# Expert loop: VectorE splits its two thirds of the next second weights one block later, GpSimd keeps its third where it was

## The chip, the cores and the metric

The program runs on one core of a Trainium2 chip. The metric is the device time of one execution in microseconds (us). The engines are TensorE (PE in the profile; its weight loads are PEld), VectorE (DVE), ScalarE (ACT), GpSimd (POOL) and SyncE (SP, which here only starts DMA). A name with q behind it (DVEq) is the sequencer of that engine: register loads, branches and semaphore work.

## The reference, cut to what matters

Three stages follow each other. A linear attention with a decaying state gives 3072 token rows of 384 numbers. A dense layer pair (384 to 2048, leaky ReLU, back to 384) works on these rows. The last stage routes each row to one of 8 experts, and this is where the change lies:

```
do_compute = x @ w_skip > 0
e_idx = np.argmax(xc @ w_gate, axis=1)
for e in range(E):
    h = np.maximum(xc[mask] @ w1[e], 0.0)       # 384 -> 1024
    y[mask] = gate_w[mask, None] * (h @ w2[e])  # 1024 -> 384
out[do_compute] = xc + y
```

Everything is float32. The kernel reaches that precision by splitting each operand of a matmul in a high part (rounded to the type that TensorE reads fast) and a low part (what is left), and by adding three products: high by high, high by low, low by high.

## The kernel before, in words

Attention and dense layers fill most of the span. Then the rows are sorted by expert into blocks of 128 rows; every expert has at least one block, and an expert's rows are padded to whole blocks. A table called `plan` holds, for each block, its expert (`EXPERT`), which half of the weight buffers that expert uses (`PARITY`), a flag `FIRST` that is 1 in the first block of an expert (but 0 for the last expert, which has no successor to prepare), the number of blocks (`TOTAL`) and where the ids of the block's rows lie (`SPOT`). Each engine runs a loop over blocks of its own, unrolled four times, and reads the table at run time into registers with `value_load`.

The order on each engine in block j, by lines of the profile:

- TensorE: transposes the hidden block j (L806), then the first product of block j+1 (L779, 18 matmuls), which needs the low rows `zt_lo` of block j+1 and the low first weights `w1_lo`; the turning of the gathered rows of block j+2 (L772), which needs their gather to have landed; two register loads (L819, L820); and the second product of block j (L825, 24 matmuls), which waits at L821 for `eht_lo` and at L822 until all three thirds of `w2_lo` of this block's expert are there.
- ScalarE: high part of the transposed hidden block (`eht_hi`, L1066, two halves); if block j+1 is the first of an expert e, the high parts of w1 of e+1 (L949, three thirds); ReLU of the hidden block j+1 (L1045, L1046); high rows of block j+2 (`zt_hi`, L1041); if block j is the first of an expert e, the high parts of w2 of e+1 (L1038, three thirds), after waiting until `w2_lo` of e is complete.
- VectorE: low part of the hidden block (`eht_lo`, L1493, two halves); if block j+1 is the first of an expert, `w1_lo` of the next expert (L1508, three thirds); low rows (`zt_lo`, L1475); if block j is the first of an expert, its two thirds of `w2_lo` of the next expert (L1522); and last the result of block j (`res`, L1528), which waits for the second product of block j and frees its PSUM bank.
- GpSimd: if block j is the first of an expert, its third of `w2_lo` of the next expert (L1629); then it waits that the output of block j-1 has been written and that `res` of block j is there, copies the ids (`put`, L1637), scatters the rows to the output (L1640), and gathers the rows of block j+4 (L1599, L1602).
- SyncE: loads the raw weights of expert e into the half that expert e-2 used. The load of w1 (L488) waits for `w1_lo` of e-2, the load of w2 (L496) for all three thirds of `w2_lo` of e-2; before it goes on to the next expert it waits until both have landed.

Within an engine the order is that of the program. Between engines only semaphores order the work. In a `value_load` of a block's flag and the two that follow if it is 1, VectorE's sequencer does nothing else, though instructions issued before may still run.

Of the kernel before, what the change touches and what calls it, by code (L numbers as in the profile page):

```python
# [17 lines left out]
ALU = mybir.AluOpType  # L18
ACT = mybir.ActivationFunctionType
AX = mybir.AxisListType  # L20
F32 = mybir.dt.float32
# [11 lines left out]
E = 8  # L33
# [15 lines left out]
EW = KT * EF  # L49
PIECES = 3  # L50
PIECE = EW // PIECES
HOTS = 8
UNROLL = 4
COLS = BLOCKS + 1 + UNROLL
# [25 lines left out]
CONSTS = ALT + E  # L80


EXPERT, PARITY, FIRST, TOTAL, SPOT = 0, COLS, 2 * COLS, 3 * COLS, 3 * COLS + 1

def build(nc, rk_t, rk_nat, v_nat, w_cols, u_rows, win, wout, wout_t, gates, experts, consts, out, z_rows):
    ctx = ExitStack()
# [4 lines left out]
    with ctx:  # L91
# [3 lines left out]
        def sem(name):  # L95
            return ctx.enter_context(nc.semaphore(name))
# [76 lines left out]
        def sb4(name, shape, dt=F32):  # L173
            return sb(name, shape, dt, moe)

        raw2 = sb4("raw2", [P, 2 * EW])
        w2_hi = sb4("w2_hi", [P, 2 * EW], F32R)
        w2_lo = sb4("w2_lo", [P, 2 * EW], F32R)
# [23 lines left out]
        plan = sb4("plan", [P, SPOT + COLS], I32)  # L202
# [88 lines left out]
        s_w2_hi = sem("w2_hi")  # L291
        s_w2_lo = sem("w2_lo")
# [21 lines left out]
        s_dve_past = sem("dve_past")  # L314
# [786 lines left out]
        def _(dve):  # L1101
# [151 lines left out]
            def linked(ins):  # L1253

                ins.then_inc(s_route, 1)
                routed[0] += 1
                dve.wait_ge(s_route, routed[0])
# [193 lines left out]
            dve.tensor_scalar(below[:], eidf[:], float(E - 2), None, ALU.min)  # L1451
            dve.tensor_copy(plan[:, TOTAL:TOTAL + 1], ends[:, E - 1:E])
            linked(dve.tensor_reduce(par[:], cmp2[:], AX.X, ALU.add))
            dve.memset(plan[:, FIRST:FIRST + 1], 1)
            dve.tensor_tensor(plan[:, FIRST + 1:FIRST + COLS], below[:, 1:], below[:, 0:COLS - 1], ALU.subtract)
            dve.tensor_copy(plan[:, PARITY:PARITY + COLS], par[:]).then_inc(s_plan_done, 1)
# [15 lines left out]
            def turned_rows(par, n):  # L1472

                dve.wait_ge(s_zt_hi, n)
                dve.tensor_tensor(zt_lo[par][:].rearrange("a k t -> a (k t)"), bank[4][:, 0:DM],  # L1475
                                  zt_hi[par][:].rearrange("a k t -> a (k t)").bitcast(F32),
                                  ALU.subtract).then_inc(s_zt_lo, 1)
# [6 lines left out]
            with dve.Fori(0, (BLOCKS + 1) // UNROLL) as jj:  # L1484
                with dve.If(UNROLL * jj < blocks):
                    for u in range(UNROLL):
                        j = UNROLL * jj + u
                        with dve.If(j < blocks):

                            for half in range(2):  # L1490
                                dve.wait_ge(s_eht_hi, 2 * j + half + 1)
                                rows = slice(4 * half, 4 * half + 4)
                                dve.tensor_tensor(eht_lo[:, rows, :].rearrange("a f t -> a (f t)"),  # L1493
                                                  bank[2 + half][:],
                                                  eht_hi[:, rows, :].rearrange("a f t -> a (f t)").bitcast(F32),
                                                  ALU.subtract).then_inc(s_eht_lo, 1)

                            first = dve.value_load(plan[0:1, bass.ds(FIRST + j + 1, 1)], min_val=0, max_val=1)
                            with dve.If(first > 0):
                                e = dve.value_load(plan[0:1, bass.ds(EXPERT + j + 1, 1)], min_val=0,  # L1500
                                                   max_val=E - 1)
                                odd = dve.value_load(plan[0:1, bass.ds(PARITY + j + 1, 1)], min_val=0,
                                                     max_val=1)
                                for i in range(PIECES):
                                    cols = bass.ds((1 - odd) * EW + PIECE * i, PIECE)
                                    dve.wait_ge(s_w1_hi, PIECES * e + PIECES + i + 1)
                                    dve.sem_inc(s_dve_past, 1)
                                    dve.tensor_tensor(w1_lo[:, cols], raw1[:, cols], w1_hi[:, cols].bitcast(F32),  # L1508
                                                      ALU.subtract).then_inc(s_w1_lo, 1)

                            with dve.If(j < blocks - 2):
                                turned_rows(u % 2, j + 3)

                            first = dve.value_load(plan[0:1, bass.ds(FIRST + j, 1)], min_val=0, max_val=1)
                            with dve.If(first > 0):
                                e = dve.value_load(plan[0:1, bass.ds(EXPERT + j, 1)], min_val=0, max_val=E - 1)
                                odd = dve.value_load(plan[0:1, bass.ds(PARITY + j, 1)], min_val=0, max_val=1)
                                for i in range(1, PIECES):
                                    cols = bass.ds((1 - odd) * EW + PIECE * i, PIECE)
                                    dve.wait_ge(s_w2_hi, PIECES * e + PIECES + i + 1)  # L1520
                                    dve.sem_inc(s_dve_past, 1)
                                    dve.tensor_tensor(w2_lo[:, cols], raw2[:, cols], w2_hi[:, cols].bitcast(F32),  # L1522
                                                      ALU.subtract).then_inc(s_w2_lo, 1)

                            spot_j = dve.value_load(plan[0:1, bass.ds(SPOT + j, 1)], min_val=0, max_val=SPOTS - 1)
                            dve.wait_ge(s_ey_done, j + 1)
                            dve.wait_ge(s_res_free, j + 1)
                            dve.scalar_tensor_tensor(res[u % 2][:], bank[5 + u % 2][:, 0:DM],  # L1528
                                                     found[:, bass.ds(spot_j, 1), 1], zg[u][:],
                                                     ALU.mult, ALU.add).then_inc(s_res_done, 1)  # L1530
# [169 lines left out]
```

## Time and profile before

| what | value |
|---|---|
| median of 3 runs | 735.33 us (731.72 to 738.29) |
| the profiled execution | 734.31 us |
| its span, first to last instruction | 732.6 us |
| TensorE busy | 689.9 us, 94% of the span |
| VectorE, ScalarE, GpSimd busy | 405.9, 307.1, 105.0 us |
| mean granted TensorE clock | 0.979 of full speed |

The span is 1.7 us shorter than the execution's time. A busy share is an average over stages; which wait counts is read stage by stage. In rows of the timeline the first number is the start in us from the beginning of the span, the second the length, and the bracket at the end, if there is one, is how long the engine stood idle before it and what ended that. The blocks are numbered from 0; the expert loop of this input has 14.

### The profile page before, as it was taken

Reading aid. Unit: us, or ns where it says so; the run is one execution under the profiler, and the core shown is the slowest. Engines: PE = TensorE matmul, PEld = TensorE weight load, DVE = VectorE, ACT = ScalarE, POOL = GpSimd, SP = SyncE. Lnnn points to the kernel's source line nnn. Section 1 sums busy time; section 2 is a strip of 40 time slices with the busy share of each in tenths; the row PEclk is TensorE's granted clock in tenths of the full one; section 3 lists DMA queues with packets and bytes.
Section 4 is the critical chain, followed back from the end, with each engine's and each line's share of the span. In section 5 each row is a group of like instructions: output and inputs, shape, how many; then the busy total and the mean of one; then the engine's idle time right before and its main releaser. Section 6 shows DMA issues by size and latency. Waiting matters only on the chain.

```text
span 732.6 us, 14146 instructions
## 1 busy us (share of the span) xinstructions
PE 689.9 (94%) x4365; PEld 650.5 (89%) x4366; DVE 405.9 (55%) x839; ACT 307.1 (42%) x665; POOL 105.0 (14%) x120
## 2 busy tenths in 40 slices
PE   7977999999999999999999999999998899998973
PEld 7877999999999999999999999999994788987773
DVE  8654565755665565466466545533557352745741
ACT  4434544333444442444443344433442453646530
POOL 6330000010010001001000100100103152344321
PEclk9998999999999999999999999999998999999997
DMA  8645342312422132242204222006015762383200
GB/s 243 200 137 193 121 132 72 99 40 59 130 65 66 36 108 59 60 130 65 66 22 118 63 60 87 12 13 235 1 62 197 285 227 106 111 293 126 100 19 8
DMA packets 38681, 77.44 MB, mean 106 GB/s; under 512 B 8568, under 2 KB 26902, under 8 KB 38624
## 3 DMA queue, kind: packets, MB, share of 16 engines
q1 hardware_dynamic: 33632, 62.37, 27.4%
q10 hardware_dynamic: 2432, 9.76, 3.6%
q0 software_dynamic: 2560, 4.58, 2.0%
q8 instruction: 32, 0.52, 0.3%
q14 instruction: 25, 0.20, 0.1%
HBM read 61.09 MB, written 12.41 MB: 100 GB/s over the span
## 4 chain that ended last, share of the span: by engine, by line
PE 84%; DVE 4%; ACT 4%; issue 4%; ACTq 1%; DVEq 1%; POOL 1%; DMA 1%; POOLq 0%; SPq 0%
PE bank L687 28%; PE bank L705 26%; PE bank L825 6%; PE bank L779 5%; PE bank L569 4%; PE bank L625 3%; PE bank L620 2%; PE bank L764 2%; PE bank L638 2%; PE bank L806 1%; PE bank L663 1%; ACT w_hi L1038 1%; PE bank L607 1%; DVE h_sb L1202 1%; ACT h_sb L920 1%
## 5 line engine op out<-in xcount | busy, mean ns | idle before, releaser
L1202 DVE TENSOR_TENSOR h_sb<-h_sb,bank 128x384 f32<-128x384 f32 x128 | 70.8, 553 | 173.3 <-ACT h_sb L920 172.9
L920 ACT ACTIVATE h_sb<-bank 128x384 f32<-128x384 f32 x128 | 62.8, 491 | 246.8 <-PE bank L687 242.8
L687 PE MATMUL bank<-x_hi,win_hi 128*128 128x384 f32 x384 | 135.6, 353 | 2.7 <-DVE win_lo L1224 1.6
L705 PE MATMUL bank<-wout_hi,g_hi 128*128 128x394 f32 x384 | 131.7, 343 | 0.0
L705 PE MATMUL bank<-wout_lo,g_hi 128*128 128x394 f32 x384 | 131.2, 342 | 0.0
L705 PE MATMUL bank<-wout_hi,g_lo 128*128 128x394 f32 x384 | 131.2, 342 | 0.0
L687 PE MATMUL bank<-x_hi,win_lo 128*128 128x384 f32 x384 | 130.5, 340 | 0.0
L687 PE MATMUL bank<-x_lo,win_hi 128*128 128x384 f32 x384 | 130.3, 339 | 0.0
L1563 POOL DMA_INDIRECT id_list<-idgate,dst x24 | 24.2, 1007 | 480.2 <-DVE dst L1307 475.3
L1209 DVE TENSOR_TENSOR g_lo<-h_sb,g_hi 128x384 fp32r<-128x384 f32 x128 | 70.9, 554 | 33.4 <-ACT g_hi L927 32.3
L927 ACT ACTIVATE g_hi<-h_sb 128x384 fp32r<-128x384 f32 x128 | 66.7, 521 | 42.9 <-DVE h_sb L1202 40.5
L687 PEld LDWEIGHTS bank<-x_hi,win_hi 128*128 128x128 f32 x384 | 72.8, 189 | 9.4 <-issue 7.0
L687 PEld LDWEIGHTS bank<-x_lo,win_hi 128*128 128x128 f32 x384 | 73.1, 190 | 0.0
L687 PEld LDWEIGHTS bank<-x_hi,win_lo 128*128 128x128 f32 x384 | 73.0, 190 | 0.0
L705 PEld LDWEIGHTS bank<-wout_hi,g_lo 128*128 128x128 f32 x384 | 72.5, 189 | 0.0
L705 PEld LDWEIGHTS bank<-wout_hi,g_hi 128*128 128x128 f32 x384 | 72.5, 189 | 0.0
L705 PEld LDWEIGHTS bank<-wout_lo,g_hi 128*128 128x128 f32 x384 | 72.4, 188 | 0.0
L877 ACT ACTIVATE am<-const,diag 128x128 f32<-128x128 f32 x168 | 53.2, 391 | 9.6 <-PE bank L625 6.0
L825 PE MATMUL bank<-w_hi,eht_hi 128*128 x112 | 40.0, 357 | 12.0 <-DVE eht_lo L1493 9.3
L825 PE MATMUL bank<-w_hi,eht_lo 128*128 x112 | 38.9, 347 | 0.0
L825 PE MATMUL bank<-w_lo,eht_hi 128*128 x112 | 38.8, 346 | 0.0
L569 PEld LDWEIGHTS bank<-rt,kb 64*128 64x128 f32 x384 | 24.4, 193 | 14.4 <-issue 11.7
(187 smaller groups left out, 993.0 us busy)
## 6 DMA issues: line engine op xcount, KB each, us to landing
raw<-in_experts SPq DMA_DIRECT2D x32, 768.0 KB, 6.1
rkt<-in_rk_t SPq DMA_DIRECT2D x46, 192.0 KB, 3.6
rkn<-in_rk_nat SPq DMA_DIRECT2D x21, 384.0 KB, 4.1
v<-in_v_nat SPq DMA_DIRECT2D x24, 192.0 KB, 2.8
z_rows<-z_sb SPq DMA_DIRECT2D x24, 192.0 KB, 2.8
out<-z_sb SPq DMA_DIRECT2D x24, 192.0 KB, 2.8
stage<-in_win ACTq DMA_DIRECT2D x4, 768.0 KB, 4.6
stage<-in_wout_t ACTq DMA_DIRECT2D x4, 768.0 KB, 6.1
```

The costliest lines, as they stand in the source:

```text
L569: mm = pe.matmul(scores_in(n)[q][:, P * p:P * p + P], kb[n % 2][rows, p, :], rt[n % 2][rows, p, :], start=True, stop=True)
L625: mm = pe.matmul(y_ps[64 * q:64 * q + 64, P * p:P * p + P], v_of(n)[:, D * h:D * h + 64], am[q][:, p, :], start=n // B == 0 and p == 0, st ...
L687: mm = pe.matmul(h_ps[t % 2][:, 0:GT], a[:, kk, cols], b[G % 2][:, kk, :], start=n == 0, stop=n == 3 * KT - 1)
L705: mm = pe.matmul(z_ps[i][:, 0:ZW], a[t % 3][:, tok], b[:, f, :], start=f == 0 and j == 0, stop=f == FT - 1 and j == 2)
L779: mm = pe.matmul(eh_ps[c][:], a[par][:, kk, :], b[:, bass.ds(base + EF * kk + 512 * c, 512)], start=kk == 0 and a is zt_hi and b is w1_hi, ...
L825: mm = pe.matmul(ey_ps[u % 2][:, 0:DM], a[:, f, :], b[:, bass.ds(odd * EW + DM * f, DM)], start=f == 0 and a is eht_hi and b is w2_hi, sto ...
L877: ins = act.activation(am_of(n)[h % 2][:, h // 2, :], ident, ACT.Copy, scale=diag_of(n)[:, h:h + 1])
L920: act.activation(h_sb[t % 2][:], h_ps[t % 2][:, 0:GT], ACT.Copy, scale=SLOPE).then_inc(s_h_scaled, 1)
L927: act.activation(g_hi[t % 3][:], h_sb[t % 2][:], ACT.Copy).then_inc(s_g_hi_done, 1)
L1202: dve.tensor_tensor(h_sb[t % 2][:], h_sb[t % 2][:], h_ps[t % 2][:, 0:GT], ALU.max).then_inc(s_leaky, 1)
L1209: dve.tensor_tensor(g_lo[t % 3][:], h_sb[t % 2][:], g_hi[t % 3][:].bitcast(F32), ALU.subtract).then_inc(s_g_lo_done, 1)
L1563: pool.indirect_dma_start(out=id_list[:, :], out_offset=bass.IndirectOffsetOnAxis(ap=dst[:, n:n + 1], axis=0), in_=idgate[:, n, :], in_off ...
```

## The change

On VectorE the low parts of w2 are no longer made at the end of the first block of an expert, between `zt_lo` and `res`, but in the block after it, right behind `eht_lo` and ahead of `w1_lo`. The flag, the expert and the parity of block j-1 are read for it. So that block 0 can read them too, one column is put ahead of the tables, and its flag is cleared by one more memset. GpSimd's third, ScalarE, TensorE and SyncE are as they were.

```diff
-EXPERT, PARITY, FIRST, TOTAL, SPOT = 0, COLS, 2 * COLS, 3 * COLS, 3 * COLS + 1
+EXPERT, PARITY, FIRST, TOTAL, SPOT = 1, COLS + 1, 2 * COLS + 2, 3 * COLS + 2, 3 * COLS + 3
...
+            dve.memset(plan[:, FIRST - 1:FIRST], 0)
             dve.memset(plan[:, FIRST:FIRST + 1], 1)
...
                                                   ALU.subtract).then_inc(s_eht_lo, 1)
+                            first = dve.value_load(plan[0:1, bass.ds(FIRST + j - 1, 1)], min_val=0, max_val=1)
+                            with dve.If(first > 0):
+                                e = dve.value_load(plan[0:1, bass.ds(EXPERT + j - 1, 1)], min_val=0, max_val=E - 1)
+                                odd = dve.value_load(plan[0:1, bass.ds(PARITY + j - 1, 1)], min_val=0, max_val=1)
+                                for i in range(1, PIECES):
+                                    cols = bass.ds((1 - odd) * EW + PIECE * i, PIECE)
+                                    dve.wait_ge(s_w2_hi, PIECES * e + PIECES + i + 1)
+                                    dve.sem_inc(s_dve_past, 1)
+                                    dve.tensor_tensor(w2_lo[:, cols], raw2[:, cols], w2_hi[:, cols].bitcast(F32),
+                                                      ALU.subtract).then_inc(s_w2_lo, 1)
 
                             first = dve.value_load(plan[0:1, bass.ds(FIRST + j + 1, 1)], min_val=0, max_val=1)
...
                             with dve.If(j < blocks - 2):
                                 turned_rows(u % 2, j + 3)
-
-                            first = dve.value_load(plan[0:1, bass.ds(FIRST + j, 1)], min_val=0, max_val=1)
-                            with dve.If(first > 0):
-                                e = dve.value_load(plan[0:1, bass.ds(EXPERT + j, 1)], min_val=0, max_val=E - 1)
-                                odd = dve.value_load(plan[0:1, bass.ds(PARITY + j, 1)], min_val=0, max_val=1)
-                                for i in range(1, PIECES):
-                                    cols = bass.ds((1 - odd) * EW + PIECE * i, PIECE)
-                                    dve.wait_ge(s_w2_hi, PIECES * e + PIECES + i + 1)
-                                    dve.sem_inc(s_dve_past, 1)
-                                    dve.tensor_tensor(w2_lo[:, cols], raw2[:, cols], w2_hi[:, cols].bitcast(F32),
-                                                      ALU.subtract).then_inc(s_w2_lo, 1)
```

## Rows read from the trace of the kernel before

**Rows 1.** Waits in the expert loop: who waited for whom, us in total, times, longest

```profile
PE bank L825 <- DVE eht_lo L1493: 9.3, 4, 5.5
PE bank L825 <- issue: 2.6, 3, 1.1
```

**Rows 2.** Timeline of TensorE, blocks 2 and 3 (start, us, line, tile)

```profile
596.91 1.04 PE L806 MATMUL bank<-const,eh 128*128 128x128 f32 x8
...
602.16 0.42 PE L825 MATMUL bank<-w_hi,eht_hi 128*128 x1
...
606.44 1.04 PE L806 MATMUL bank<-const,eh 128*128 128x128 f32 x8
```

**Rows 3.** Timeline of TensorE, the second product where it waited

```profile
592.62 0.44 PE L825 MATMUL bank<-w_hi,eht_hi 128*128 x1 [1.21 <-DVE eht_lo L1493]
...
612.49 0.44 PE L825 MATMUL bank<-w_hi,eht_hi 128*128 x1 [0.55 <-issue]
...
642.10 0.44 PE L825 MATMUL bank<-w_hi,eht_hi 128*128 x1 [0.77 <-DVE eht_lo L1493]
...
662.37 0.44 PE L825 MATMUL bank<-w_hi,eht_hi 128*128 x1 [1.01 <-issue]
...
694.35 0.43 PE L825 MATMUL bank<-w_hi,eht_hi 128*128 x1 [1.81 <-DVE eht_lo L1493]
...
715.95 0.68 PE L825 MATMUL bank<-w_hi,eht_hi 128*128 x1 [5.54 <-DVE eht_lo L1493]
```

**Rows 4.** Timeline of VectorE, expert loop

```profile
608.14 1.29 DVE L1493 TENSOR_TENSOR eht_lo<-bank,eht_hi 128x512 fp32r<-128x512 f32 x2 [0.75 <-ACT eht_hi L1066]
...
618.51 1.29 DVE L1493 TENSOR_TENSOR eht_lo<-bank,eht_hi 128x512 fp32r<-128x512 f32 x2 [0.80 <-ACT eht_hi L1066]
621.68 3.57 DVE L1508 TENSOR_TENSOR w_lo<-raw,w_hi  x3 [1.88 <-ACT w_hi L949]
...
634.59 0.55 DVE L1475 TENSOR_TENSOR zt_lo<-bank,zt_hi 128x384 fp32r<-128x384 f32 x1
...
687.74 4.61 DVE L1522 TENSOR_TENSOR w_lo<-raw,w_hi  x2 [2.97 <-ACT w_hi L1038]
...
714.43 1.27 DVE L1493 TENSOR_TENSOR eht_lo<-bank,eht_hi 128x512 fp32r<-128x512 f32 x2
```

**Rows 5.** VectorE's w2_lo instructions (ns: least, median, most; first and last start)

```profile
L1522 DVE TENSOR_TENSOR w_lo<-raw,w_hi x14: 1211/1222/3476, 587.0 to 712.8; - x14
```

**Rows 6.** Timeline of ScalarE, blocks 1 and 13

```profile
587.40 1.06 ACT L1066 ACTIVATE eht_hi<-bank 128x512 fp32r<-128x512 f32 x2
...
710.83 1.06 ACT L1066 ACTIVATE eht_hi<-bank 128x512 fp32r<-128x512 f32 x2
```

**Rows 7.** VectorE's sequencer in block 1, a flag that is 0: load begun, code behind the branch

```profile
L1498 DVEq FUSED_REGOPS  x2: 57/124/190, 589.2 to 589.7; - x2
...
L1511 DVEq ALU_OP  x1: 40/40/40, 590.2 to 590.2; - x1
```

**Rows 8.** Timeline of TensorE, first product beside the VectorE row of 634.59

```profile
636.62 0.71 PE L779 MATMUL bank<-w_hi,zt_hi 128*128 x2
```

**Rows 9.** Timeline of GpSimd, block 7

```profile
660.84 1.15 POOL L1637 COPY put<-id_put 128x1 uint32 x1 [6.06 <-issue]
...
665.07 0.98 POOL L1602 DMA_INDIRECT zg<-z_rows,get  x1 [0.81 <-POOL get L1599]
```

**Rows 10.** Timeline of SyncE, load of w1 of expert 7

```profile
664.24 0.83 SPq L488 DMA_DIRECT2D raw<-in_experts  x2
```

**Rows 11.** Granted clock of a stretch (us, PE busy, clock, DMA share, GB/s)

```profile
695.50:698.40 2.90, 2.90 (x11) 0.50 0.18 68
```

**Rows 12.** Chain of waits, the second products of blocks 9 and 11

```profile
673.23 4.43 PE bank L825 x24
...
694.35 5.99 PE bank L825 x24
```

**Rows 13.** Timeline of TensorE, an idle stretch earlier in the kernel

```profile
46.39 0.41 PE L687 MATMUL bank<-x_hi,win_hi 128*128 128x384 f32 x1 [1.65 <-DVE win_lo L1224]
```

## The prediction, made before the changed kernel was run

> **What bounds the kernel now.** I read the page first: TensorE is busy 94% of the span, and the change touches only the expert loop, from 576 us on. There I asked who makes TensorE wait. Two kinds of wait appear [rows 1]: four times for `eht_lo`, 9.3 us in all, and three times for "issue", 2.6 us in all. Then the timeline of each engine by blocks. An unhindered block takes 9.53 us: 5.25 from its first transpose to its second product, 4.28 from there to the next transpose [rows 2]. The second product is where all waits end [rows 3]. The bracket there is 0.25 short of the true delay, since the records of the transposes before it overlap its start: block 3's product should start at 606.44 + 5.25 = 611.69 and starts at 612.49, 0.80 late with a bracket of 0.55. So the second products are late by 1.46 in block 1, 0.80 in block 3, 1.02 in block 6, 1.26 in block 8, 1.32 in block 9 (a bracket of 1.07, the largest of the three), 2.06 in block 11 and 5.8 in block 13.
>
> VectorE's `w2_lo` pieces run in blocks 0, 1, 5, 6, 9, 10 and 12, 14 instructions in all [rows 5], and `w1_lo` in 0, 4, 5, 8, 9 and 11. Read with the program, experts 0 to 7 have 1, 4, 1, 3, 1, 2, 1 and 1 blocks. This decides the case: where an expert has one block (0, 2, 4, 6), the next expert's w2 is needed in the very next block.
>
> The waits for `eht_lo` come from the place of the old split. In block 10 VectorE idles 2.97 for ScalarE's high parts and then takes 4.61 for two pieces [rows 4], so that `res` and the next `eht_lo` come late, and TensorE stops 1.81. The pieces themselves vary: 1.21 us alone, up to 3.48 beside GpSimd's third [rows 5].
>
> **What the change removes.** `res` and `eht_lo` no longer stand behind the split. `eht_lo` then starts 1.70 after the first transpose (606.44 and 608.14 [rows 2, 4]), or 0.63 after ScalarE's `eht_hi` where ScalarE is late. The pieces no longer run beside GpSimd's third, so I take 1.2 each, as the three `w1_lo` pieces in 3.57 [rows 4], not the 3.48 end; that end would add 2.3 to each block in which they are needed at once. The trace shows the slow pieces exactly where both engines split. The Trainium skill (SBUF — State Buffer, Who interferes with whom) has an instruction with two SBUF inputs and any GpSimd instruction that reads SBUF exclude each other for the whole instruction; by that GpSimd's short id copies could still hold up a piece, by 0.2 each, and the sum would be up to 0.8 higher.
>
> **What it adds.** Behind `eht_lo` now stand three register loads, then the pieces. The nearest row is `w1_lo` in the same place: `eht_lo` starts at 618.51, the first piece at 621.68, 3.16 later [rows 4], the same in five of its six cases within 0.1. So two pieces end 3.16 + 2.4 = 5.6 after `eht_lo`'s start, and TensorE starts 0.25 later (714.43 + 1.27 to 715.95 [rows 4, 3]): 5.85. The bounds of the 3.16: part of it may be ScalarE's own w1 split, which comes as late; with no sequencer time at all it would be `eht_lo`'s 1.27. I take 3.16, because the loads are the same three.
>
> In an unhindered block `w2_lo` is ready 1.70 + 5.85 = 7.55 after the first transpose, and TensorE wants it at 5.25. So **each block that needs it at once is late by 2.3 or more**. These are blocks 1, 6, 10 and 13.
>
> **Block by block**, new start against old, in this trace's time.
> - Block 1: `eht_hi` at 587.40 [rows 6] as before, `eht_lo` 588.03, product 593.88 against 592.62 [rows 3]: +1.26.
> - Block 3: the 0.80 there was no compute wait. GpSimd's writes and gathers queue behind SyncE's weight loads. In block 7 it stood 6.06 for the write of block 6, `put` came at 660.84, and the gather for block 11 at 665.07, just behind the load of w1 of expert 7 at 664.24 [rows 9, 10]. With the split out of the way the gathers leave a little earlier or as before, the loads of w2 (which wait for `w2_lo`) 3 to 5 later, and TensorE wants the rows later. I take all three of these waits as gone: block 3 stands at +0.46.
> - Block 6: `eht_lo` 637.57 + 0.47 = 638.04, product 643.89 against 642.10: +1.79.
> - Block 8: less 1.26: +0.54. Block 9: less 1.32: -0.78.
> - Block 10: transposes at 673.23 - 0.78 + 4.28 = 676.7, `eht_lo` 1.70 to 1.8 later at 678.5 (ScalarE has just finished its w2 split), product 684.35 against 682.76: +1.6.
> - Block 11: two of the next expert's pieces, not needed at once. The old delay of 2.06 goes: -0.46. In the old trace the clock then stood at 0.50, that is 1.2 of 2.4 GHz [rows 11], and the product took 5.99, not 4.43 [rows 12]. Without the idle time this 1.54 goes: -2.0.
> - Block 12: VectorE had `w2_lo` of 6 ahead of `w1_lo` of 7. Transposes of block 11 at 684.35 + 4.28 = 688.6, `eht_lo` 690.35, pieces 693.5 to 695.95, `w1_lo` until 699.5, `zt_lo` 700.05; the first product of block 13 wants them at 698.96 and starts at 700.3. So 1.3 is given back: -0.67.
> - Block 13: ScalarE's `eht_hi` 710.83 - 0.67 = 710.16, `eht_lo` 710.79, product 716.64 against 715.95: **+0.7**, which goes to the end.
>
> Four blocks cost, four give, and the sum is +0.7. The loads of w2 move by 3 to 5 us, but their data is used 20 us or more later, so ScalarE doesn't wait. In blocks where the flag is 0 the check still costs 589.2 to 590.15, 0.95 [rows 7], now ahead of `w1_lo`: in block 5 `zt_lo` ends at 635.14 + 0.95, and 0.25 later is 636.34, against a first product at 636.62 [rows 4, 8]. Hidden, with 0.3 to spare; blocks 4 and 9 have 0.2. If that cover goes, each costs some tenths. GpSimd's queue gains: its third no longer meets VectorE's, and `res` is earlier. The memset of one column costs between 0 and a third's 1.2 [rows 5]; near 0 for one column, and TensorE runs filler matmuls there.
>
> **The clock.** The new idle stretches in blocks 1, 6 and 10 are 2.4 to 2.5 us long by bracket. After one of 1.81 the clock fell [rows 3, 11, 12]; after 1.65 and 1.21 it did not [rows 13, 3]. One fall costs 1.54. I take two falls of the three: +3.1. All three would be 4.6, none 0. Block 13 falls in both.
>
> The sum: 734.31 + 0.7 + 3.1 = 738.1. The profiled execution is 1.0 under the median of the three runs, which span 6.6 us; carried to the median it is 739. I say **738.5**.
>
> **Rivals.**
> - A, the loads don't count. If the sequencer runs through its loads while `eht_lo` works, the pieces start up to 1.9 sooner, the four blocks lose nearly nothing, block 12 doesn't wait, no clock falls. Against it: the 3.16 in rows of the same form. The time: 734.3 + 0.7 - 4 x 1.9 = 727.4. Chance 0.06.
> - B, as forecast, but no clock fall in the three stretches, because 2.4 is not long enough at the moment it falls in, or `w2_lo` somewhat sooner: 732 to 736. For it: only one stretch of 1.81 is a thin base. Chance 0.24.
> - C, slower. The transfers meet again: the load of w2 of expert 4 now starts about 605.6, and the gather for block 5 leaves at 604; the loads of w2 of 6 and w1 of 7 start about 655.6 and 667 and the gathers for 10 and 11 leave at 654 and 662 to 667. If a gather lands only behind the whole load, the three waits stay, 3.4 in all. It decides from the point where the gather leaves later than the load. With three falls of the clock: 734.3 + 0.7 + 4.6 + 3.4 = 743.0. Chance 0.15.
>
> That the change doesn't do what it says I see no way for: the tables are shifted as a whole and block 0 reads a cleared flag.
>
> **How the numbers follow.** My forecast (736 to 741) has 0.55. The range 733.5 to 743 leaves out A, the lowest of B and the end of C. What a measurement can tell from no change is 1%, 7.35 us: faster than 728.0 is A, 0.05; slower than 742.7 is most of C, 0.12; within it 0.83.
>
> **What would show it.** Right: VectorE's `w2_lo` pieces at 1.2 us in blocks 1, 2, 6, 7, 10, 11 and 13, about 3.2 behind `eht_lo`'s start; TensorE waits at the second products of 1, 6, 10 (2.4 each) and 13 (about 7), none in 11; short or no waits in 3, 8 and 9; a wait of 1.3 at the first product in block 12; ScalarE's w2 split where it was. Wrong: pieces less than 2.5 behind `eht_lo`'s start (A), "issue" waits in 3, 8 and 9 (C), or a full clock behind the three long waits (B).

## The result

| | before | changed |
|---|---|---|
| median of 22 runs each | 736.99 us | 740.05 us |
| lowest, highest | 731.31, 748.91 | 735.83, 752.85 |
| profiled execution, span | 732.6 us | 738.2 us |

The ratio of the changed kernel to the one before is 1.0071, 95% interval 1.0049 to 1.0093: slower by 0.7%, within the 1% that the prediction counted as no change; the median of 740.05 lies inside its range. All ratios here leave out executions in the chip's slower state, in which one runs some per cent longer at a lower granted clock, while the medians are of all executions, so the two can differ (the medians alone give 1.0042). The changed kernel was run once more beside the later experiments: 1.0038, 1.0006 to 1.0070.

**The profile after.** First the page, then who waited for whom in the expert loop [rows 1].

```profile
PE 692.6 (94%) x4365; PEld 653.4 (89%) x4366; DVE 400.9 (54%) x840; ACT 308.0 (42%) x665; POOL 103.5 (14%) x120
```

```profile
PE bank L825 <- DVE w_lo L1508: 12.5, 4, 6.8
...
PE bank L779 <- DVE zt_lo L1476: 1.6, 1, 1.6
```

VectorE is busy 5 us less (its `w2_lo` pieces no longer meet GpSimd's third), and TensorE waits longer. The four waits for `eht_lo` of before [rows 1] are now four waits for the split itself (L1508 in this kernel), 12.5 us in place of 9.3. The second products where TensorE waits, and the one first product [rows 3]:

```profile
597.55 0.43 PE L825 MATMUL bank<-w_hi,eht_hi 128*128 x1 [2.30 <-DVE w_lo L1508]
...
647.44 0.43 PE L825 MATMUL bank<-w_hi,eht_hi 128*128 x1 [1.77 <-DVE w_lo L1508]
...
687.80 0.43 PE L825 MATMUL bank<-w_hi,eht_hi 128*128 x1 [1.64 <-DVE w_lo L1508]
...
704.23 0.73 PE L779 MATMUL bank<-w_hi,zt_hi 128*128 x2 [1.60 <-DVE zt_lo L1476]
...
720.46 0.68 PE L825 MATMUL bank<-w_hi,eht_hi 128*128 x1 [6.78 <-DVE w_lo L1508]
```

These are blocks 1, 6, 10, 12 and 13. VectorE in blocks 1, 11 and 13 [rows 4]:

```profile
591.78 1.29 DVE L1494 TENSOR_TENSOR eht_lo<-bank,eht_hi 128x512 fp32r<-128x512 f32 x2 [1.08 <-ACT eht_hi L1066]
595.04 2.36 DVE L1508 TENSOR_TENSOR w_lo<-raw,w_hi  x2 [1.98 <-issue]
...
697.01 2.36 DVE L1508 TENSOR_TENSOR w_lo<-raw,w_hi  x2 [1.96 <-issue]
700.03 3.50 DVE L1521 TENSOR_TENSOR w_lo<-raw,w_hi  x3 [0.65 <-issue]
...
714.70 1.29 DVE L1494 TENSOR_TENSOR eht_lo<-bank,eht_hi 128x512 fp32r<-128x512 f32 x2 [1.10 <-ACT eht_hi L1066]
717.95 2.36 DVE L1508 TENSOR_TENSOR w_lo<-raw,w_hi  x2 [1.96 <-issue]
```

The pieces start 3.25 behind `eht_lo`'s start (595.04 - 591.78, 717.95 - 714.70), and in between VectorE is idle 1.96 and waits for nothing but its own sequencer ("issue"). Two pieces take 2.36 to 2.43 in all seven blocks; before they took 2.36 in blocks 1 and 6 and 3.35 to 4.61 in the other five [rows 4, 5].

The code ahead of the loop is the same but for one memset of 0.06 us, yet its time is not: the first transpose of block 0 comes at 576.09 in the trace before and at 579.84 after.

```profile
579.84 1.09 PE L806 MATMUL bank<-const,eh 128*128 128x128 f32 x8 [0.85 <-ACT eh L1046]
```

In twelve of the thirteen traces of this study it lies between 576.1 and 584.0, in the thirteenth (TensorE's loads first) at 593.8. The changed kernel was behind long before the memset: the first instruction that fills the table, at 560.3 before, came at 564.2, and from 40 to 80 us, far ahead of any changed code, the granted clock was 0.87 before and 0.79 after:

```profile
40.00:80.00 40.00, 34.25 (x224) 0.87 0.38 125
```

```profile
40.00:80.00 40.00, 32.73 (x191) 0.79 0.37 119
```

(Columns: us, TensorE busy, granted clock, DMA share, GB/s.) So these 3.75 us are no effect of the change, and everything below is counted from that transpose. Each number of the table is the start of a block's second product less the start of the first transpose of block 0 in the same trace:

| block | before | changed | difference | forecast |
|---|---|---|---|---|
| 1 | 16.53 | 17.71 | +1.18 | +1.26 |
| 3 | 36.40 | 36.77 | +0.37 | +0.46 |
| 6 | 66.01 | 67.60 | +1.59 | +1.79 |
| 8 | 86.28 | 86.65 | +0.37 | +0.54 |
| 9 | 97.14 | 96.19 | -0.95 | -0.78 |
| 10 | 106.67 | 107.96 | +1.29 | +1.6 |
| 11 | 118.26 | 117.48 | -0.78 | -0.46 |
| 12 | 129.09 | 128.62 | -0.47 | -0.67 |
| 13 | 139.86 | 140.62 | **+0.76** | **+0.7** |
| end of the last product | 145.76 | 147.67 | +1.91 | |

The forecast of block 13 counts on the kernel before having lost 1.54 to the clock in block 11 [rows 11, 12] and the changed one not, and in these two traces that is so.

The last step is the clock: the last product took 7.05 us, before 5.90, since the clock was at half for longer. Of the two rows, with the same columns, the first is the wait ahead of it, the second the product.

```profile
713.00:720.00 7.00, 0.68 (x7) 0.71 0.02 5
720.46:727.60 7.14, 7.04 (x24) 0.60 0.00 0
```

The waits of blocks 1, 6 and 10 were not followed by a fall in this execution.

### The profile page after: what moved, and what is told of

Its sections match the earlier page's. It is cut to its first block, busy times and chain, and to the rows that moved or that the text cites. A ratio compares the mean times of both kernels' runs of the same rounds, so it can differ in the third digit from the quotient of the medians.

```text
span 738.2 us, 14148 instructions
## 1 busy us (share of the span) xinstructions
PE 692.6 (94%) x4365; PEld 653.4 (89%) x4366; DVE 400.9 (54%) x840; ACT 308.0 (42%) x665; POOL 103.5 (14%) x120
## 4 chain that ended last, share of the span: by engine, by line
PE 82%; ACT 4%; DVE 4%; issue 4%; DVEq 2%; ACTq 2%; POOL 1%; DMA 0%; POOLq 0%; SPq 0%
PE bank L687 28%; PE bank L705 26%; PE bank L825 6%; PE bank L779 4%; PE bank L569 4%; PE bank L625 3%; PE bank L620 2%; PE bank L764 2%; PE bank L638 2%; PE bank L663 1%; PE bank L806 1%; ACT w_hi L1038 1%; PE bank L607 1%; DVE w_lo L1508 1%; DVE h_sb L1202 1%
## 5 line engine op out<-in xcount | busy, mean ns | idle before, releaser
L825 PE MATMUL bank<-w_hi,eht_hi 128*128 x112 | 39.8, 356 | 12.5 <-DVE w_lo L1508 12.5
```

The costliest lines, as they stand in the source:

```text
L825: mm = pe.matmul(ey_ps[u % 2][:, 0:DM], a[:, f, :], b[:, bass.ds(odd * EW + DM * f, DM)], start=f == 0 and a is eht_hi and b is w2_hi, sto ...
```

## The experiments

Each was compared with the kernel before on its own chip; the median of before was 736.33, 737.81 and 736.73 us in the three groups. "Late" is how much more than 5.25 us lies between a block's first transpose and its second product. All rows of the table are from one trace each.

| kernel | late in block 1, 3, 6, 8, 9, 10, 11, 13 | last product | first transpose to end | ratio to before, 95% interval |
|---|---|---|---|---|
| before | 1.42, 0.80, 1.02, 1.26, 1.32, 0.01, 2.07, 1.33 | 5.90 | 145.76 | 1 |
| changed | 2.55, 0.01, 2.25, 0, 0.01, 2.25, 0.01, 2.56 | 7.05 | 147.67 | 1.0071 (1.0049 to 1.0093) |
| changed, again | 2.56, 0.01, 2.24, 0.01, 0.01, 2.25, 0.01, 2.55 | 6.44 | 148.61 | 1.0038 (1.0006 to 1.0070) |
| two more loads | 3.80, 0.01, 3.47, 0.01, 0.13, 3.47, 0.01, 3.99 | 6.63 | 158.65 | 1.0149 (1.0102 to 1.0197) |
| filled waits | 2.54, 0, 2.24, 0.01, 0.01, 2.25, 0.01, 2.56 | 4.43 | 145.04 | 0.9982 (0.9942 to 1.0023) |
| late weight loads | 1.41, 1.80, 1.02, 1.37, 0.53, 0.50, 1.49, 1.34 | 5.99 | 145.59 | 1.0014 (0.9959 to 1.0069) |
| TensorE's loads first | 1.41, 0, 1.01, 0, 1.44, 1.02, 0.05, 1.32 | 6.36 | 141.73 | 0.9950 (0.9907 to 0.9994) |
| only where not urgent | 1.36, 1.22, 1.02, 2.38, 1.32, 1.06, 0.05, 1.32 | 6.10 | 148.88 | 1.0076 (1.0043 to 1.0109) |
| GpSimd last third | 0.16, 1.32, 2.19, 0, 0.01, 2.16, 0.04, 0 | 6.86 | 142.53 | 0.9973 (0.9936 to 1.0009) |
| the same, filled | 0.20, 1.28, 2.17, 0, 0, 2.16, 0, 0 | 4.45 | 139.53 | 0.9957 (0.9922 to 0.9993) |
| res first | 0.86, 0.01, 0.51, 0.01, 0.01, 0.51, 0.01, 0.83 | 6.41 | 138.43 | **0.9909** (0.9879 to 0.9939) |
| res first, filled | 0.88, 0.01, 0.53, 0.01, 0.01, 0.51, 0.53, 0.81 | 4.43 | 137.29 | 0.9917 (0.9878 to 0.9956) |
| res first, loads first, filled | 0.86, 0, 0.51, 0, 0, 0.55, 0.12, 0.86 | 4.43 | 136.62 | **0.9891** (0.9830 to 0.9952) |

In block 13 there is no first product, and "late" there is the part beyond 5.25 of a stretch whose own work is only 1.0; 0 there means no later than 5.25. Waits in other blocks are named in the text. The trace of "TensorE's loads first" is of its longest execution (747.98 us), with most of the loss ahead of the loop.

**Two more loads: is the sequencer the price of the new place?**

```diff
 odd = dve.value_load(plan[0:1, bass.ds(PARITY + j - 1, 1)], min_val=0, max_val=1)
+for i in range(2):
+    dve.value_load(plan[0:1, bass.ds(PARITY + j - 1, 1)], min_val=0, max_val=1)
```

> The changed kernel with two more register loads of the same kind (their values unused) between the three that are there and VectorE's w2_lo pieces. My theory: the loads are the price of the new place. A load takes 0.7 to 0.75 us of VectorE's sequencer, so the pieces start 4.7 instead of 3.25 behind eht_lo's start, the second products of blocks 1, 6, 10 and 13 and the first product in block 12 start 1.45 later each, and the time is the changed kernel's plus 5 x 1.45 = 7.2 us, less what clock falls do: about 12 above the kernel before. Rival, the loads run beside eht_lo and cost nothing: pieces still 3.25 behind, no change against the changed kernel.

The median was 747.62 us. VectorE in block 1:

```profile
589.48 1.29 DVE L1494 TENSOR_TENSOR eht_lo<-bank,eht_hi 128x512 fp32r<-128x512 f32 x2 [1.08 <-ACT eht_hi L1066]
593.99 2.36 DVE L1510 TENSOR_TENSOR w_lo<-raw,w_hi  x2 [3.22 <-issue]
```

The pieces start 4.51 behind `eht_lo`, not 3.25: two loads cost 1.25, and TensorE is 1.2 to 1.4 later in each of blocks 1, 6, 10 and 13, and 1.5 later at the first product in block 12. So the loads are on the path one by one, and the rival is out. All three longer waits (brackets of 3.59, 3.22 and 2.83) were now followed by a fall; their products took 6.01, 5.94 and 6.02 in place of 4.43:

```profile
596.49 0.43 PE L825 MATMUL bank<-w_hi,eht_hi 128*128 x1 [3.59 <-DVE w_lo L1510]
```

The last product starts at 152.02; less the 4.7 of the falls that is 6.7 above the changed kernel, with 7.2 forecast.

**Filled waits, and the changed kernel again: what does the clock cost?**

```diff
+if u == 1:
+    with pe.If(jj < 1): fill(1)
+    with pe.If(jj > 2): fill(6)
+if u == 2:
+    with pe.If(jj > 0): fill(1)
 cur = pe.value_load(plan[0:1, bass.ds(EXPERT + j, 1)], ...)
```

where `fill(n)` is n times `pe.matmul(bank[7][:], ident, const[:, 0:4 * P], ...)`.

> The changed kernel with filler matmuls (ident by const, into bank 7, their result unused) ahead of the second product where it waits: one of 1.05 us in blocks 1, 6 and 10, six in block 13. The starts of the products stay as they are (the filler is shorter than the wait). My theory: the clock is what is left of the change beside the 0.8 us by which the product of block 13 starts later; in the profiled execution only the last product ran slow, 7.05 against 4.44, so it gains 2.6 there, and in other executions also 1.5 for each fall after the waits of 1, 6 and 10: 3 to 5 us below the changed kernel, so about even with the kernel before. Rival, falls are not caused by these waits: no gain against the changed kernel.

> The changed kernel once more on the chip of these runs, for the filled version to be compared with, and for a second profiled execution. My theory: 5 us above the kernel before by the ratio, the product starts in the loop as in the first profile within 0.3, and some of the waits in blocks 1, 6 and 10 (1.6 to 2.3 by bracket) followed by a fall of the clock that costs 1.5. Rival: no fall after any of the three again, and the difference to before is only 2.

The second round of the changed kernel was 2.8 us above before by its ratio, where 5 was forecast and 2 was the rival's number. The filled kernel's median was 735.70, the changed one's 740.35 on the same chip: 4.7 us less, by the ratios 4.1, though their intervals overlap. In the traces, from the first transpose to the end, it is 2.6 and 3.6 (145.04 against 147.67 and 148.61). The starts are those of the changed kernel to 0.02 us, the last one at 140.61 against 140.62; only the clock differs, and the last product took 4.43. The second execution of the changed kernel shows the other part. In block 6, after the same wait as in the first, its product took 6.00 in place of 4.43:

```profile
651.60:657.60 6.00, 6.00 (x26) 0.72 0.90 279
```

So one fall among six such waits in two executions, and a longer half-speed stretch at the end (7.05 and 6.44 against 5.90). The +0.76 of the table is not the price of the new place: the trace of the kernel before holds a fall in block 11 (5.99 in place of 4.43) and a slow last product (5.90), together 3.0. Less these its loop would take 142.7, and the changed kernel at full clock takes 145.0. By this estimate the new place costs 2.3, and the clock took about as much from the changed kernel (2.6 and 3.6) as from the one before (3.0). How often a fall comes in the other executions was not seen, since they have no trace.

**Late weight loads: were the waits of blocks 3, 8 and 9 behind SyncE's loads?**

```diff
 sp.wait_ge(s_w2_lo, PIECES * (e - 1))
+after_block = {3: 1, 4: 2, 5: 6, 6: 7, 7: 10}
+if e in after_block:
+    sp.wait_ge(s_ey_done, after_block[e] + 1)
 load_w2(e)
```

> The kernel before, with SyncE's loads of w2 of experts 3 to 7 held back until the second product of block 1, 2, 6, 7 or 10 is done, about where the changed kernel starts them; VectorE is as before. My theory: the three waits that the changed kernel lost at the second products of blocks 3, 8 and 9 (0.80, 1.26, 1.32) were gathers and row writes behind these loads, so they go here too, with everything else as before: 3.4 us faster than before, product starts of blocks 4 to 8 earlier by 0.8, of 9 by 2.1, of 10 on by 3.4. Rival, the waits went because GpSimd was freed from VectorE's split or because TensorE came later: then the brackets at blocks 3, 8 and 9 stay and the time is that of before.

Measured 740.66, a ratio of 1.0014, where 3.4 us less was forecast. The waits of blocks 3 and 8 did not go:

```profile
618.69 0.44 PE L828 MATMUL bank<-w_hi,eht_hi 128*128 x1 [1.55 <-issue]
...
669.67 0.44 PE L828 MATMUL bank<-w_hi,eht_hi 128*128 x1 [1.12 <-issue]
```

Block 3 got later by 1.0 and block 8 by 0.1, new waits of 0.96 and 0.50 came up in blocks 7 and 10, and block 9's shrank from 1.32 to 0.53. But the test does not decide whether the loads count, for held back they met the same gathers again. Block 3's gather left at 609.16 and was issued by 610.14, with loads of w1 and w2 at 608.64 and 611.90 on either side, and TensorE could go on behind its rows only at 616.4:

```profile
611.90 0.80 SPq L496 DMA_DIRECT2D raw<-in_experts  x2
```

```profile
609.16 0.98 POOL L1605 DMA_INDIRECT zg<-z_rows,get  x1 [0.82 <-issue]
```

What goes with the waits is when the rows have landed. In the kernel before, the gathers for blocks 3, 8 and 9 landed 5.6, 5.7 and 5.3 after the end of their issue, each with a weight load issued 0.8 to 3.1 ahead of it; of the others in the loop the slowest took 3.2. They landed 4.05, 4.62 and 4.70 behind the first transpose of the block that turns them. The second product started 1.9 to 2.0 later, behind TensorE's two register loads. For block 9, the landing (from 665.07 on) and the first of the two loads:

```profile
DMA to landing us min/median/max: 6.3/6.3/6.3
```

```profile
L819 PEldq TENSOR_LOAD <-plan x1: 302/302/302, 671.5 to 671.5; - x1
```

How early the gather leaves is the other half. The end of its issue lies ahead of the first transpose of the block by (block 3, 8, 9): before 1.55, 1.09, 0.61; late loads 1.50, 0.68, 1.69; changed 2.50, 3.57, 3.60; res first 3.06, 2.79, 2.58. Neither half is enough alone. In the kernel before, blocks 2 and 7 had only 0.72 and 0.60 and no wait, as these gathers landed in 2.7 and 3.2. In the changed kernel, TensorE could go on behind the rows of blocks 3 and 8 only 5.5 and 5.2 after the end of the issue, so the gathers were about as slow as before, but had left early enough.

**TensorE's loads first: what is it that waits there?**

```diff
+cur = pe.value_load(plan[0:1, bass.ds(EXPERT + j, 1)], min_val=0, max_val=E - 1)
+odd = pe.value_load(plan[0:1, bass.ds(PARITY + j, 1)], min_val=0, max_val=1)
 with pe.If(j < blocks - 2):
     pe.wait_ge(rows_in[(u + 2) % UNROLL], 16 * (jj + 1 + (u + 2) // UNROLL))
     turn_rows((u + 2) % UNROLL)
-cur = pe.value_load(plan[0:1, bass.ds(EXPERT + j, 1)], min_val=0, max_val=E - 1)
-odd = pe.value_load(plan[0:1, bass.ds(PARITY + j, 1)], min_val=0, max_val=1)
```

> The kernel before, with TensorE's two register loads for the second product put ahead of its wait for the gathered rows, not behind it. My theory for the waits of blocks 3, 8 and 9: the rows land late enough to hold TensorE's sequencer, though its queue still has the first product to work on, and then the two loads, 0.8 us each, stand bare in front of the second product. So these three starts come back to 5.3 behind the first transpose (before 6.05, 6.51 and 6.57), or, where the rows are later than the queue, keep a rest of at most 0.5; blocks 1, 6, 11 and 13 stay as they are: 3 us below the kernel before. Rival, the rows themselves are late: the same waits remain, now ahead of the turning of the rows.

In blocks 3 and 8 the second product follows the turned rows at once, with the gathers as late as before (1.49 and 1.14 ahead):

```profile
629.17 0.49 PE L772 MATMUL bank<-const,zg 128*128 128x128 f32 x3
629.41 0.42 PE L826 MATMUL bank<-w_hi,eht_hi 128*128 x1
```

So there the rows were in time for TensorE's array, but not for its sequencer: it stood at the semaphore, and the two loads came bare behind it. Block 9 keeps its wait, and now the trace names it:

```profile
688.72 0.55 PE L772 MATMUL bank<-const,zg 128*128 128x128 f32 x3 [1.23 <-DMA zg<-z_rows,get]
```

Its gather left 0.72 behind the first transpose, 1.3 later than before, and in this kernel the rows really are late. In the kernel before they landed at 4.70, ahead of the turning at 5.01, and block 9 had the same reason as 3 and 8.

The kernel is 0.5% faster than before, 2.8 us in the medians, with 3 forecast, but not by the forecast alone. Blocks 3 and 8 gave 2.1. Against the forecast block 11 did not stay: its delay went from 2.07 to 0.05, its fall of the clock (1.6) with it, and block 10 got 1.0 later.

**Only where not urgent: the gain without the loss?** The table got two flags, NOW (the expert has one block) and LATER (it has more); VectorE checks LATER of j-1 in the new place and NOW of j in the old.

```diff
-first = dve.value_load(plan[0:1, bass.ds(FIRST + j - 1, 1)], ...)   # new place
+first = dve.value_load(plan[0:1, bass.ds(LATER + j - 1, 1)], ...)
...
+first = dve.value_load(plan[0:1, bass.ds(NOW + j, 1)], ...)         # old place
+with dve.If(first > 0):
+    ...
```

> Two flags in the table in place of one: where the expert has one block, so that the next w2 is needed in the next block, VectorE splits in the old place; where it has more (experts 1, 3 and 5 here), in the new place. My theory: the changed kernel loses only in blocks 1, 6, 10 and 13; here these are as in the kernel before, and what it won stays: block 11's delay of 2.06 less 1.3 given back in block 12, its clock fall of 1.5, and the waits of blocks 3, 8 and 9, 3.4. Together 2 to 5.5 below the kernel before, I say 4. Rival, the clock decides and not the place: no more than 1 away from before.

It is slower than before: 741.43, 1.0076. Block 11's delay went as forecast, but `eht_lo` of blocks 4, 8 and 12 came late, 2.70, 5.15 and 1.71 for "issue", and with it the first products in blocks 5 and 9 (1.2 and 1.3 late) and the second of block 8 (2.4). The first product in block 12 was 2.0 late.

```profile
671.56 1.29 DVE L1504 TENSOR_TENSOR eht_lo<-bank,eht_hi 128x512 fp32r<-128x512 f32 x2 [5.15 <-issue]
```

All three are the first blocks of a new round of the unrolled loop. In block 8 VectorE's sequencer takes the branch back at 665.9 and runs its next instruction at 671.2:

```profile
L1495 DVEq COMPARE_BRANCH  x1: 63/63/63, 665.9 to 665.9; - x1
L1495 DVEq FUSED_REGOPS  x1: 58/58/58, 671.2 to 671.2; - x1
```

The queue that brings instructions moved 20 packets in the loop, where the kernels before and changed each moved 6 (queue, packets, MB, share; first this kernel, then the changed one):

```profile
q14 instruction: 20, 0.16, 0.3%
```

```profile
q14 instruction: 6, 0.05, 0.1%
```

The likeliest reading is that the loop's code, longer by one split, had to be fetched at each round, behind weight loads; which engine's the 20 packets were the trace doesn't say. It agrees with the Trainium skill (Runtime: NRT & Kernel Launch, Instruction fetch mechanics): a taken branch out of the pages at hand forces a fetch by DMA. That the fetch caused the stop is not shown. The idea as such is not refuted; in this form it costs more than it brings.

**GpSimd takes the last third: was it the old place, or the meeting in it?**

```diff
-for i in range(1, PIECES):               # VectorE, old place
+for i in range(PIECES - 1):
...
-cols = bass.ds((1 - odd) * EW, PIECE)    # GpSimd
-pool.wait_ge(s_w2_hi, PIECES * e + PIECES + 1)
+cols = bass.ds((1 - odd) * EW + PIECE * (PIECES - 1), PIECE)
+pool.wait_ge(s_w2_hi, PIECES * e + PIECES + PIECES)
```

> The kernel before, with VectorE's split in its old place, but GpSimd takes the last third of w2 and VectorE the first two. My theory: in the kernel before VectorE's first piece waited until GpSimd's had ended (587.00 + 2.49 against 586.01 + 2.40), so the old place lost to the meeting, not to its position. Now VectorE is two thirds on before GpSimd's begins: pieces of 1.2 us, second products of blocks 1, 6 and 11 at most 0.3 late (before 1.4, 1.0, 2.1), no clock fall in 11, block 13 1.4 earlier, the row waits in 3, 8 and 9 gone or shorter as put and gather leave earlier: 6 to 10 us below the kernel before, I say 8. Rival, order decides and not the meeting (res and eht_lo still stand behind the pieces): no more than 2 below before.

Little of it came: 1.9 us in the medians where 8 was forecast, which is also what the rival allowed (no more than 2), and a ratio of 0.9973 that is not clear of 1. Blocks 1, 11 and 13 do as forecast (0.16, 0.04 and 0 late). Block 3 kept its wait (1.32) and block 7 got one of 0.69. Blocks 6 and 10 got worse, 2.2 late, as in the blocks ahead of them (5 and 9) the two met again. VectorE, then GpSimd, in block 9:

```profile
679.35 4.56 DVE L1522 TENSOR_TENSOR w_lo<-raw,w_hi  x2 [1.59 <-ACT w_hi L1038]
```

```profile
680.11 2.71 POOL L1629 TENSOR_TENSOR w_lo<-raw,w_hi  x1 [4.23 <-ACT w_hi L1038]
```

VectorE's first piece ended about 680.57 (1.22 after its start), GpSimd was waiting since 680.11 and went first, until 682.82, and VectorE's second ended at 683.91. In the other blocks VectorE's second piece had begun or ended before GpSimd asked. So the place and the meeting are not fully parted by this run; blocks 1, 11 and 13 show that without a meeting the old place holds up next to nothing. The Trainium skill's rule of an exclusive lock, first come first served (SBUF — State Buffer, Who interferes with whom), gives just this order.

> The kernel with GpSimd's third last, and four filler matmuls ahead of the second product of the last block, 4.2 us of the 4.5 to 5 that it waits there. My theory: the last product runs at the full clock, 4.4 and not 5.9 to 6.4: 1.5 to 2 below the kernel without the filler. Rival: the last wait is too short for a fall there anyway, no difference.

With four fillers in the last block (same edit as above, `fill(4)` for u == 1 and jj > 2) the last product took 4.45, not 6.86, and the ratio was 0.9957. The medians of the two kernels differ by 2.3 us, with 1.5 to 2 forecast.

**Res first: keep the block, change only what stands behind the split.**

```diff
 first = dve.value_load(plan[0:1, bass.ds(FIRST + j, 1)], ...)
 with dve.If(first > 0):
     e, odd = ...
+    spot_j = ...; wait for ey_done, res_free; res
     for i in range(1, PIECES):
         ...                               # w2_lo, as before
-spot_j = ...; wait for ey_done, res_free; res
+with dve.If(first < 1):
+    spot_j = ...; wait for ey_done, res_free; res
```

> The kernel before, with VectorE's w2_lo pieces in the same block but behind res, not ahead of it, and the register loads ahead of the wait for the second product. My theory: the pieces still wait for GpSimd's third (the first of VectorE's two ends 1.1 after GpSimd's ends), so only the 0.55 of res leaves the way of eht_lo, in blocks 1, 6, 11 and 13: 1.5 to 2 below before, plus what earlier row writes give. Against the new place of the changed kernel it saves the loads: product starts of blocks 1, 6 and 13 about 1.3 to 2 earlier than there. Rival, the sequencer's loads don't count: then it is no better than the changed kernel.

The best single edit: 729.98, 0.9909. In blocks 1, 6, 10 and 12 the register loads now run while VectorE waits for the second product anyway (in 0, 5 and 9 `res` still stands idle 2.1 to 2.6 for "issue"). GpSimd's third is nearly over when VectorE starts: two pieces take 2.36 to 3.13, and 3.55 in block 12 (before 2.36 to 4.61). The row waits are gone, with `res`, `put` and the gathers earlier. TensorE and VectorE in block 1:

```profile
592.21 0.44 PE L825 MATMUL bank<-w_hi,eht_hi 128*128 x1 [0.65 <-DVE eht_lo L1493]
```

```profile
587.77 0.62 DVE L1521 SCALAR_TENSOR_TENSOR res<-bank,found,zg 128x384 f32<-128x384 f32 x1 [2.56 <-issue]
588.31 2.46 DVE L1528 TENSOR_TENSOR w_lo<-raw,w_hi  x2
590.69 1.28 DVE L1493 TENSOR_TENSOR eht_lo<-bank,eht_hi 128x512 fp32r<-128x512 f32 x2
```

It brought 6.4 us where 1.5 to 2 were expected: I had left the meeting with GpSimd in place and counted the row waits as lucky extras. In the traces the last product starts 7.8 earlier: 3.4 of it are the waits of blocks 3, 8 and 9, 1.6 the fall in block 11 that this execution did not have, and the rest is `eht_lo` coming sooner.

> VectorE's split behind res, and four filler matmuls ahead of the second product of the last block. My theory: starts as with res first alone (the last product 132.0 after the first transpose of block 0), the last product 4.4 and not 6.4: 2 us below that kernel, so 1.2% below the kernel before. Rival: no fall without the filler in most executions, no difference.

> Split behind res, TensorE's loads ahead of the rows, filler in the last block. My theory: with res first the row waits are already gone (gathers leave 2.6 to 3.1 ahead of the transposes that need them, before 0.6 to 1.6), so the loads' new place adds nothing and the time is that of the filled version within 0.3%. Rival: a little of the wait was left and it is 1 us faster.

Both show the last product at 4.43. The 2 us forecast for the filler are not in the times. Their medians are 730.93 and 728.77, their ratios 0.9917 and 0.9891; against 0.9909 without the filler none of the three can be told from another. In the traces the three end 138.4, 137.3 and 136.6 after the first transpose.

## Why the prediction was right, and where it was not

**Where the product starts: right, step by step.** The forecast start of the last product was +0.7, measured +0.76 in one execution, and the same in two more once the single fall is taken out (140.61 in the filled kernel, and 142.17 - 1.57 = 140.60). It holds only against a kernel before whose clock fell in block 11, as in its one trace; whether it does so in most executions was not seen. The price of the new place, 3.16 from `eht_lo` to the pieces, measured 3.25; the two added loads show that it is sequencer time. The pieces at 1.2 us came true in all seven blocks, block 11's delay and its fall went, and block 12 gave back 1.6 at its first product where 1.3 was forecast.

**A small cover went.** I had left 0.2 to 0.3 us between `zt_lo` and the first product of blocks 6 and 10. In the profiled execution one register load of VectorE took 0.94 us where the median is 0.30, while GpSimd was issuing a gather, and `w1_lo` of block 9 came 0.66 later than forecast (of block 5, 0.54):

```profile
L1515 DVEq TENSOR_LOAD <-plan x1: 941/941/941, 675.5 to 675.5; - x1
```

```profile
675.74 0.99 POOL L1604 DMA_INDIRECT zg<-z_rows,get  x1 [0.81 <-issue]
```

The first product was 0.24 and 0.36 late. It cost nothing, as the second product waited for `w2_lo` anyway; it only split that wait in two, which is why its bracket reads 1.77 and 1.64 and not the 2.4 of my text.

**The row waits of blocks 3, 8 and 9: right in size, wrong in reason.** They went, as forecast. But "the loads of w2 3 to 5 later" is not why, or only in part. In all three blocks a gather that took over 5 us beside a weight load held TensorE's sequencer, and two register loads stood exposed behind it (for blocks 3 and 8 the loads-first kernel shows it; for block 9 the kernel before's own trace, 671.36 and 671.5). In the changed kernel the gathers of blocks 3 and 8 were about as slow and met the loads again, as rival C had said; but they left 0.95 and 2.5 sooner before the block that needs them, since `res` no longer stood behind VectorE's split and TensorE came later. Only in block 9 did the load move out of the way: the load of w1 of expert 7 left at 670.59, and the gather issued until 667.18 had landed in 2.1. What the later loads alone are worth stays open, since the late-loads kernel put them beside the gathers again. Rival C was wrong in its end, not in its meeting.

**The clock: too high, and partly in the wrong place.** I took two falls of 1.54 after the waits of blocks 1, 6 and 10. The two traces show none and one. What I had left out is the last product: block 13 "falls in both", but the stretch at half speed got longer, and the product by 1.15 and 0.54. Together that is 1.15 in one trace and 2.1 in the other, where 3.1 was forecast. The waits alone are not enough to say when a fall comes: the bracket of 2.30 in block 1 had none in two executions, 1.77 in block 6 had none, and about the same wait (1.87) in the second had one; 3.59, 3.22 and 2.83 had three of three. The filled waits put the clock's whole share in the changed kernel at 2.6 and 3.6 by the traces and at 4.1 by the ratios; in the kernel before it was not measured alone (its one trace holds a fall in block 11 and one at the end, 1.5 each).

**The total.** Forecast +3.8 us on the profiled execution (0.7 and 3.1); the loop of the two traces gives +1.9 and +2.9, the ratios give +5.2 (3.6 to 6.9) and +2.8 (0.4 to 5.2). That the medians moved by 3.1 and the forecast by 3.2 (735.33 to 738.5) is in part luck, as the forecast of the clock was too high for both traces. The difference between traces and ratios I can't assign: one candidate is block 11 of the kernel before, whose fall (1.5) the forecast counts as won and which may be missing in many executions, and what happens ahead of the loop moves a single execution by more than that.

## What to carry to other kernels

When work is moved to where its input is ready, count the register loads that come with it: here three of them, 0.6 to 0.7 us each, cost more in blocks 1, 6, 10 and 13 than the stall they replaced, and the same work behind another instruction of the old place hides most of them under a wait that is there anyway. A semaphore wait ahead of register loads exposes the loads even when the data is in time; load first, then wait. When rows come late, look at when they landed: here it took a late start and a slow transfer together. And before a split is moved to make two engines not meet, ask who else stands behind it: the result and the gathers behind VectorE's split were worth 3.4 us here.

## What the runs showed that I had not expected

- In the kernel whose loop grew by one more `If` block VectorE's sequencer stood for up to 5.3 us at the branch back, with 20 instruction packets in place of 6.
- A chain of two pieces on VectorE can lose its turn to GpSimd in the middle: the same swap freed blocks 1 and 13 of nearly all their wait (1.42 and 1.33 to 0.16 and 0) and cost blocks 6 and 10 1.2 us and 2.2 us.
- A register load of VectorE took 0.83 and 0.94 us beside GpSimd's issue of a gather, where the median is 0.30; in the kernel before one of TensorE's took 0.82 at 654.4, beside the gather issued from 653.79 on. That one caused the other is not shown; in the filled version the same blocks had no late first product.
